# The MLP stage's normalization as scale and shift on ScalarE in place of VectorE

## The reference, cut to what matters

```python
# 1: a causal convolution over 7 tokens with softmax weights per head
# 2: Fourier mixing and an MLP
mixed = real(fft(fft(x, axis=1), axis=2))
u  = x + mixed
mu = mean(u, axis=-1);  var = mean((u - mu) ** 2, axis=-1)
un = (u - mu) / sqrt(var + 1e-6)            # <- the normalization
x  = u + relu(un @ w_ch1) @ w_ch2
# 3: phase mixing over all 4224 tokens
theta = x @ w_theta
y = w_tok_r @ (x * cos(theta)) + w_tok_i @ (x * sin(theta))
u = x + y
out = u + relu(u @ w_ch)
```

## Time and profile before

| | |
|---|---|
| Median of three runs | 3316.98 us (3311.91 to 3325.58) |
| The profiled execution | 3315.71 us |
| Its span, from first to last instruction | 3313.6 us |
| Mean granted TensorE clock over the span | 0.962 |
| Busy over the span: TensorE | 2993.9 us (90%) |
| VectorE | 2691.4 us (81%) |
| GpSimd | 1549.1 us (47%) |
| ScalarE | 1245.2 us (38%) |

### The profile page before, as it was taken

One profiled execution on the slowest core, in us unless ns is written; L12 is line 12 of the kernel. 1 busy time (PEld: TensorE's weight loads), 2 busy tenths in 40 slices (PEclk: granted clock), 3 DMA queues, 4 the chain that ended last, 5 costly groups with the idle time before them and its releaser, 6 DMA issues.

```text
span 3313.6 us, 57585 instructions
## 1 busy us (share of the span) xinstructions
PE 2993.9 (90%) x17218; PEld 2826.7 (85%) x17218; DVE 2691.4 (81%) x4407; ACT 1245.2 (38%) x2320; POOL 1549.1 (47%) x1494
## 2 busy tenths in 40 slices
PE   3555678999999799999999999999999999999999
PEld 3444327888888689999999999999999999999999
DVE  9999457999999878887878788787878788787776
ACT  1111224555555533333333333333333333333443
POOL 5666204666666544444534454444434444453221
PEclk8777899999999999999999999999999999999999
DMA  6565562323233455665656556565656556565432
GB/s 212 199 215 189 155 244 70 118 96 120 97 109 126 143 203 216 219 220 203 229 204 227 214 213 228 209 224 206 222 207 225 213 211 227 214 222 188 141 136 75
DMA packets 212231, 612.11 MB, mean 185 GB/s; under 512 B 15824, under 2 KB 59152, under 8 KB 212080
## 3 DMA queue, kind: packets, MB, share of 16 engines
q1 hardware_dynamic: 202928, 597.41, 50.4%
q10 hardware_dynamic: 9152, 12.98, 1.4%
HBM read 393.66 MB, written 216.66 MB: 184 GB/s over the span
## 4 chain that ended last, share of the span: by engine, by line
PE 66%; DVE 11%; issue 8%; POOLq 6%; DVEq 3%; DMA 2%; ACT 2%; POOL 1%; ACTq 1%; SPq 0%
PE banks L1486 54%; PE banks L1353 7%; POOLq L981 5%; DVE un L793 3%; DVE zl L748 2%; DVE angle L736 2%; DVE wl L743 1%; PE banks L1414 1%; DMA fraw<-f_low 1%; DVEq L735 1%; DVEq L718 1%; POOL head L979 1%; PE banks L1565 1%; DVE angle L733 1%; PE banks L1428 1%
## 5 line engine op out<-in xcount | busy, mean ns | idle before, releaser
L1486 PE MATMUL banks<-zh,wh 128*128 128x384 f32 x3828 | 1296.1, 339 | 58.1 <-DVE rbuf L805 58.1
L1486 PE MATMUL banks<-zh,wl 128*128 128x384 f32 x3828 | 1283.3, 335 | 0.0
L1486 PE MATMUL banks<-zl,wh 128*128 128x384 f32 x3828 | 1282.8, 335 | 0.0
L805 DVE TENSOR_TENSOR rbuf<-rbuf,banks 128x384 f32<-128x384 f32 x1168 | 643.0, 551 | 271.5 <-PE banks L1486 235.7
L1486 PEld LDWEIGHTS banks<-zh,wh 128*128 128x128 f32 x3828 | 721.2, 188 | 79.8 <-DVE rbuf L805 53.5
L1486 PEld LDWEIGHTS banks<-zl,wh 128*128 128x128 f32 x3828 | 721.4, 188 | 0.0
L1486 PEld LDWEIGHTS banks<-zh,wl 128*128 128x128 f32 x3828 | 720.9, 188 | 0.0
L1013 POOL TENSOR_TENSOR wsum<-wraw 128x384 f32<-128x384 f32 x176 | 179.0, 1017 | 1139.9 <-DVE wl L743 1014.5
L1182 ACT ACTIVATE wh<-wsum 128x384 fp32r<-128x384 f32 x704 | 370.2, 526 | 787.3 <-PE banks L1486 741.1
L743 DVE TENSOR_TENSOR wl<-wsum,wh 128x384 fp32r<-128x384 f32 x664 | 535.4, 806 | 44.9 <-ACT wh L1182 23.4
L1182 ACT ACTIVATE wh<-wraw 128x384 fp32r<-128x384 f32 x528 | 278.4, 527 | 496.5 <-PE banks L1486 496.5
(11 more groups left out here) (140 smaller groups left out, 4250.3 us busy)
## 6 DMA issues: line engine op xcount, KB each, us to landing
wraw<-w_pairs SPq DMA_DIRECT2D x176, 768.0 KB, 6.7
rbuf<-y_scr SPq DMA_DIRECT2D x176, 768.0 KB, 5.7
y_scr<-rbuf SPq DMA_DIRECT2D x160, 768.0 KB, 4.0
xin<-x_pad SPq DMA_DIRECT2D x22, 1728.0 KB, 8.1
z_scr<-zsc SPq DMA_DIRECT2D x33, 768.0 KB, 3.4
zraw<-z_scr SPq DMA_DIRECT2D x33, 768.0 KB, 7.4
x_scr<-x1s SPq DMA_DIRECT2D x22, 576.0 KB, 4.8
t_scr<-tst ACTq DMA_DIRECT2D x44, 288.0 KB, 5.8
```

The costliest lines, as they stand in the source:

```text
L805: dve.tensor_tensor(part, part, dst(k, i), ALU.add).then_inc(r_done, 1)
L1486: last = pe.matmul(dst, l[w][:, q, :], r[par][:, operand, q, :], start=starts and q == 0 and t == 0, stop=q == 2 and t == 2, skip_group_ch ...
```

## The change

The normalization (u - mu) * rstd becomes u * rstd + (-mu * rstd). VectorE writes -mu into a new tile `shift_u` of 128 x 4 beside `ve`. GpSimd multiplies it by `rstd` after Newton, with one more drain ahead, and signals `rstd_ready` from there. ScalarE then does four activations with the function Identity, with `rstd` as scale and `shift_u` as bias, at the end of its step, behind the sines. VectorE's four instructions go. Before it writes `ve` and `shift_u`, VectorE now waits for `un_ready` of the tile before, since ScalarE reads `shift_u`.

```diff
@@ allocations
         rstd = alloc(C, "rstd", [P, B])
+        shift_u = alloc(C, "shift_u", [P, B])
         newton = alloc(C, "newton", [P, B])
@@ VectorE, step_c
                         dve.drain()
+                        wait(dve, un_ready, n + 2)
                         dve.tensor_scalar(ve[:], mv[:, :, 1], 1e-6, None, ALU.add)
+                        dve.tensor_scalar(shift_u[:], mv[:, :, 0], -1.0, None, ALU.mult)
...
                 if live(n):
                     add_x2(n, s, 0)
-                if live(n + 2):
-                    dve.wait_ge(rstd_ready, n + 3)
-                    wait(dve, ut_ready, n + 2)
-                    for b in range(B):
-                        last = dve.tensor_scalar(un[:, b, 0:D], tile(s + 2)[:, b, :], mv[:, b, 0:1],
-                                                 rstd[:, b:b + 1], ALU.subtract, ALU.mult)
-                    last.then_inc(un_ready, 1)
@@ GpSimd, step_c
-                        last = pool.tensor_tensor(rstd[:], rstd[:], newton[:], ALU.mult)
-                        if newton_step < 2:
-                            pool.drain()
-                    last.then_inc(rstd_ready, 1)
+                        pool.tensor_tensor(rstd[:], rstd[:], newton[:], ALU.mult)
+                        pool.drain()
+                    pool.tensor_tensor(shift_u[:], shift_u[:], rstd[:], ALU.mult).then_inc(rstd_ready, 1)
@@ ScalarE, step_c
                 if live(n - 2):
                     sines(n)
+                if live(n + 2):
+                    act.wait_ge(rstd_ready, n + 3)
+                    wait(act, ut_ready, n + 2)
+                    for b in range(B):
+                        last = act.activation(un[:, b, 0:D], tile(s + 2)[:, b, :], ACT.Identity, bias=shift_u[:, b:b + 1],
+                                              scale=rstd[:, b:b + 1])
+                    last.then_inc(un_ready, 1)
```

## The result

The changed kernel takes 3290.19 us (median of 4 runs, 3287.56 to 3293.02) against 3316.4 us for the kernel before in the same set (3311.91 to 3325.58). The ratio is 0.9914, 95% interval 0.9897 to 0.9931. The medians themselves differ by 26.2 us and 3290.19 lies just inside the range, so the range was missed by less than the interval (3282.8 to 3294.1). The gain is larger than forecast in two more kernels whose MLP stage works like the changed one: their ratios are 0.9917 and 0.9914. The profiled execution took 3287.56 us, 28.15 less than before.

What follows compares the result with a forecast made beforehand. TensorE's own work was taken as the bound once its wait for x2s goes. −20.2 − 1.0 − 0.6 − 0.5 = −22.3 us on the profiled 3315.71 gives 3293.4; the median, 1.3 higher, gives 3295 us; range 3289 to 3309.

Steps and rivals of the forecast that it cites:

- (a): MLP loop: normalization leaves VectorE's queue, TensorE's wait for x2s goes; 20.2 us over 24 steps, 1.0 more from VectorE's stalls.
- The far end: Steps 30 and 31 of the MLP stage: VectorE gains 2 us, ScalarE's later ReLU costs 1.3; −0.5 us taken.
- (b): ScalarE in each MLP step: four added ACTIVATE take 1.75 us and delay the first ReLU by 0.3; cost 0.
- (c): GpSimd after Newton: one more drain and one 128x4 multiplication, about 0.35 us, hidden behind the sines; cost 0.
- (d): VectorE in each MLP step: one added 128x4 tensor_scalar of 0.1 us and a wait for un_ready; cost 0.
- the cover: Slack behind ScalarE's ReLU until TensorE wants hl at its fifth up-projection block: 2.7 us.
- The slower rival: Late rstd holds ScalarE's ReLU and TensorE: first loss at 4.6 us later, +33 us, 3350; chance 0.05.
- (e): Ends of the MLP stage; its first normalization goes from 2.70 us to 1.75 plus 0.35 on GpSimd: −0.6 us.
- Unknown: 16 bytes more of SBUF move buffers behind them, the Fourier stage's included: 0, between −2 and +4 us.
- Part of the gain: Rival: busier ScalarE fills the path again, gain 11 us instead of 22, 3306; chance 0.18.
- The whole 3.8 us: Rival: each step loses the normalization's full time on the chain of waits, 91 us, 3226; chance 0.02.
- no effect: Rival: TensorE's wait for x2s is really one for the down-projection; gain near 0, 3317; chance 0.03.

Runs made afterwards that it cites:

- old addresses: The changed kernel with shift_u allocated behind the Fourier stage's buffers, so that these lie where they lay before: 3289.83 us, ratio 0.9917.

## Why the prediction was right, and where it was wrong

**The bound, the step, the saving in it: right.** TensorE at 17.79 us a step, which I took from two early transposes, is what the loop now runs at, and (a)'s slack for the sum is as worked out (ready 1.4 us into the step, wanted at 2.3). The steps 2 to 31 gave 22.6 us in the two traces; my terms for them sum to 21.7. The far end was sized too small: steps 30 and 31 gave 1.2 us, forecast 0.5. ScalarE there:

```profile
1059.64 1.85 ACT L1221 ACTIVATE un<-UR,shift_u,rstd 128x192 f32<-128x192 f32 x4
1061.39 0.58 ACT L1191 ACTIVATE hh<-banks 128x512 fp32r<-128x512 f32 x1
```

The ReLU follows the normalization at once, as feared, but VectorE no longer was as late either.

**Costs of (b), (c), (d): zero, right; the cover, wrong.** The price of the ACTIVATE was 0.53 us (taken 0.5), no table was loaded in the loop, shift_u was early. But I named hl as what comes due first behind ScalarE's ReLU, with 2.7 us of cover. It is twice_x2, with 1.1. I had listed it as queued behind and not asked when TensorE wants it. That the cost came out as zero was in part luck: the ReLU is 0.2 us later than before, well within 1.1, but with the added work doubled a step lost 0.7. The slower rival's first loss at 4.6 us was wrong for the same reason.

**(e), the first normalization:** 1.86 us, and 0.3 us gained up to TensorE's first up-projection matmul, forecast 0.6.

```profile
495.98 1.86 ACT L1221 ACTIVATE un<-UR,shift_u,rstd 128x192 f32<-128x192 f32 x4 [17.96 <-POOL shift_u L1040]
```

**The step that failed: the size of the saving, taken from one trace, and the stages behind put at nothing.** The terms for the MLP stage, 20.2 + 1.0 + 0.5 = 21.7 us, were read off one trace, and the stages behind "should only shift". The one term for chance, "Unknown: 0, between −2 and +4", left 2 us of room on the good side. Two things were left out, and a third was chance.

1. The MLP stage of the first trace (619.8 us) was a good execution of it. The second trace of the same program shows 625.0, the one with an unused tile 624.0; the changed kernel, that with old addresses and that with three operations added show 598.5 to 598.7. The stage's gain is 21.2 us in the pair of traces of the result and 26 and 25 against the other two, 24.3 on the mean of three. Two things make the difference. The normalization can jump by 1.8 us a step; with it on ScalarE all 132 activations of it take the same time, so that is gone. And TensorE's granted clock can fall to 0.50 behind a wait of 2 to 3 us, which costs about 1.6 us each time. That is not gone: the changed kernel has it in its last step, where the first trace before had the same wait and kept its clock. By the traces the change removes the waits for x2s behind which the clock could fall. That it narrows the spread of the times is not shown: in one set the kernel before ran between 3311.24 and 3331.13 us (23 runs) and the changed one with old addresses between 3286.91 and 3293.68 (6 runs), but in another set nine runs of the kernel before lie within 6.8 us.
2. The product was 2.3 us shorter in the pair, 1.6 on the mean of three traces before and of the changed kernel and that with old addresses. Three times in it, at ends of the product's loops, VectorE pauses for 2.9 to 3.5 us and TensorE then waits 1.6 to 2.2 us for it. Behind some of these waits the granted clock falls. At the first and third of them, in the kernel before and then in the changed one:

```profile
1718.70:1722.10 3.40, 3.40 (x13) 0.50 0.45 181
2469.70:2473.10 3.40, 3.40 (x12) 0.51 0.27 107
```

```profile
1693.60:1697.00 3.40, 3.40 (x13) 0.51 0.47 184
2442.60:2446.00 3.40, 3.40 (x19) 1.00 0.67 256
```

The kernel before has two such stretches, the changed one has one. Over the whole product TensorE spent 3.0 us less at the lower clock (27.5 instead of 30.5), worth 1.5 us, and stood idle for 0.9 us less: together 2.4. All fourteen traces fit this. With two such stretches at the three loop ends the product took 2182.4 to 2184.6 us (five traces, all with the normalization on VectorE), with one 2181.7, 2181.8 and 2182.7 (and 2186.0 in the kernel with eight more ACTIVATE, where TensorE stood idle for 3 us more), with none 2179.3 to 2180.5 (the four more ACTIVATE, six Newton steps, the three kernels with three operations added). VectorE's program has a part in it: TensorE's three waits sum to 5.9 to 6.1 us in the five traces whose VectorE instructions are those of the kernel before (once in another order), and to 4.8 to 5.1 in the other nine. What of the program decides it is open: its length does not, since the changed kernel with three operations added has as many as the kernel before. Open too is at which wait the clock falls: in the second trace of the kernel before it fell behind one of 1.96 us and not behind one of 2.00.

VectorE's waits by releaser must not be read for this. Between 1600 and 2500 us, for the kernel before and the changed one:

```profile
DVE rbuf L805 <- issue: 22.6, 72, 3.4
```

```profile
DVE rbuf L801 <- issue: 14.8, 69, 3.2
```

It looks as if 8 us were gone in the changed kernel. But two of its three long waits, 2.97 and 2.94 us, are only put down to TensorE instead of "issue"; all three together are 9.1 us long, before 10.1.

3. The Fourier stage's 4 us in the two traces are taken as chance, and worth nothing in the medians.

On the means, 24.3 of the MLP stage, 1.6 of the product and 0.2 ahead of the stage make 26 us, where the measured ratios say 27.5 to 28.5 and the medians of the result 26.2. What is left is within the spread of the traces.

**The rivals.** "Part of the gain": did not happen. "Slower" was 4 us of GpSimd work away (3357.69 us with six Newton steps). "The whole 3.8 us" and "no effect" are excluded by the trace. The mechanism that I only read off the trace, VectorE and GpSimd shutting each other out, is shown by the addition moved ahead of Newton: the same operations on the same engines, and 1.25 instead of 3.80 us.

## What to carry to other kernels

When work leaves an engine, count the gain by the wait that it ends on the bounding engine, and find a step in the trace that happens to run without that wait: its length is the forecast. For each instruction queued behind an added one, write down when its reader wants it; the first due date counts, not the one with the most obvious reader. Before moving VectorE's scalar operations to another engine, look at what GpSimd runs beside them: reordering GpSimd's queue may give the same, and where the two meet, take the time from several executions, since it comes in stairs. Look at the granted clock behind each long wait of TensorE, in both traces, before a difference of 1 to 3 us is put down to the change.

## What the runs showed of the hardware that was not expected

Three VectorE operations of 0.17 us each in a step, 0.2 us with their overlap, made the kernel before 0.38% slower (1.0025 to 1.0050). In six steps the start of one GpSimd operation lay 0.36 us later against VectorE's, and each time a normalization fell behind one more GpSimd operation of 1.85 us. By the Trainium skill, "SBUF — State Buffer", section "Who interferes with whom", issue order decides who blocks. The traces agree where the order is clear, and show besides how a run of short operations fares against GpSimd's back to back: one gets through for each GpSimd operation. The third normalization ends 0.12 us behind the first multiplication (654.57 and 654.45), and the fourth waits for the whole second one (656.35 and 656.24).

TensorE's waits of 2.4 us for x2s cost more than their length: behind five of the seven of them the granted clock fell from 1.00 to 0.50 for a stretch, 565.8 to 569.2 us in the second trace of the kernel before, which made the step about 1.6 us longer. At the wait of 3.0 us for theta in the last step it fell in nine of the twelve traces that have this wait, and in neither of the two in which the angle came first and the wait was 0.78 us.
